# A turn in front of TensorE's first loop that jumps over the loop's code, in a chained attention and mixture-of-experts kernel

## The chip, the cores and the metric

The kernel runs on one core of a Trainium2 chip. The metric is the device time of one execution in microseconds (us). The kernel before took 394.88 us in the median of three executions (394.24 to 397.09).

## The reference

All of it is float32. Three stages stand behind one another, on 4 batches x 8 heads x 768 tokens x 48 dimensions.

```python
# 1: linear attention with decay w and bonus u, token by token
for t in range(S):
    cur = np.einsum('bhd,bhe->bhde', u[None] * kt, vt)
    y[:, :, t] = np.einsum('bhd,bhde->bhe', rt, state + cur)
    state = w[None, :, :, None] * state + np.einsum('bhd,bhe->bhde', kt, vt)
# 2: soft mixture of experts on x = y, tokens x (H*D) = 3072 x 384; 8 experts with 4 slots each
logits = x @ phi
d = softmax(logits, over tokens); slot_input = d.T @ x
slot_out[e] = relu(slot_input[e] @ w1[e]) @ w2[e]
x = softmax(logits, over slots) @ slot_out
# 3: out = relu(x @ w_in) ** 2 @ w_out, with 384 -> 2048 -> 384
```

## The kernel before, in words

The attention is cut into 24 units: 6 chunks of 128 tokens (CH = 6) by 4 pairs of heads (HP = 4), and each unit holds 4 batches. A unit is computed in matrix form: scores of keys against queries (`unit_scores`, L1005), the part of y that comes from the carried state (`unit_carried`, L1028), the part that comes from the unit's own values (`unit_own`, L1043), the step of the state (`unit_state`, L1016), the turning of the next unit's keys (`turn_keys`, L993) and of an earlier unit's x (`turn_x`, L987). The dispatch of stage 2 (`pair_logits` L973, `token_logits` L980, `turn_peaks` L1111, `spread_peaks` L1117, `gather` L1123) stands between the units' steps.

TensorE runs these units in one loop, `with pe.Fori(0, CH) as c` (L1154), whose body is written out for the 4 units of a chunk. Its order is by hand: the own part of the unit before, scores, the first half of carried, the state's step for the next unit, the second half of carried, the turning of the next keys, the turning of the x of three units ago. The other engines (VectorE is DVE, ScalarE is ACT, GpSimd is POOL, and SP issues every data transfer) have the 24 units written out without a loop. All order between engines goes by semaphores.

Ahead of the loop TensorE does this. It waits for the identity matrix and does 7 dummy products (`keep_awake`, L1130). It waits for the powers of the decay from DVE and turns them (16 small products, L1138, into `x_ps` and `kt_ps`), does 7 more dummy products, then waits for the first keys, turns them (L993) and makes the first unit's step of the state (L1016). The turned powers are needed by DVE (`kn_pow`, L729), then by POOL, which multiplies the keys with them (`keys_n`, L450), and these keys are what TensorE turns next.

Behind the loop come the experts (L1256, L1280) and then the third stage, whose products (L1320, L1340) take more than half of the time.

## Time and profile before

| | |
|---|---|
| median of three executions | 394.88 us |
| lowest, highest | 394.24, 397.09 us |
| the profiled execution | 395.28 us |
| its span, first to last instruction | 393.6 us |
| TensorE busy in the span | 382.6 us, 97% |
| VectorE, ScalarE, GpSimd busy | 250.9, 205.3, 43.9 us |
| mean granted TensorE clock | 0.991 |

The profiled execution's own time is 1.7 us longer than its span, since the span leaves out what lies ahead of the first and behind the last recorded instruction. The profile counts a busy PE by matmuls whose ends are modelled. Every float32 product that the program names once is recorded as two matmuls with two weight loads (a transpose as one of each), so a step of 16 products is a row of 32. Time in which an engine waited for nothing that the profile shows is called "issue". The queues of kind "instruction" bring the engines' own code.

### The profile page before, as it was taken

The page shows a single profiled execution, that of the slowest core. Times are in us where ns is not written, and L with a number is a line of the kernel's source. Part 1 is how long each engine was busy: PE and PEld are TensorE (multiplying, and loading weights), DVE is VectorE, ACT ScalarE, POOL GpSimd, SP SyncE. Part 2 cuts the span into 40 slices and gives each one's busy share as a digit, 9 for nine tenths or more (in the row PEclk, how much of TensorE's full clock was granted, in tenths as well). Part 3 has the DMA queues.
Part 4 walks back from the last instruction along what each step waited for, and adds up shares of the span by engine and source line. Part 5 has one row for each costly group of instructions (what it writes and reads, how often), then busy time and mean ns, then how long its engine had stood idle before and what let it go on. Part 6 is the DMA issues. An engine that isn't in the chain of part 4 may idle for free.

```text
span 393.6 us, 13159 instructions
## 1 busy us (share of the span) xinstructions
PE 382.6 (97%) x5308; PEld 337.6 (86%) x5308; DVE 250.9 (64%) x437; ACT 205.3 (52%) x378; POOL 43.9 (11%) x87
## 2 busy tenths in 40 slices
PE   7878999999999999999999999999999999999996
PEld 7667878787887533799999999999999999999996
DVE  8563887787775650498866656665666566666662
ACT  7432455655654320687665556555655565555552
POOL 7512314333310110000000000000000000000000
PEclk9996999999999999999999999999999999999999
DMA  4564799999995989800002001100200020002002
GB/s 120 179 207 159 268 300 301 295 313 299 302 358 171 378 296 408 314 0 2 0 2 80 2 0 42 38 0 0 80 0 0 0 80 0 0 0 82 0 0 82
DMA packets 29351, 50.75 MB, mean 129 GB/s; under 512 B 4112, under 2 KB 23568, under 8 KB 28944
## 3 DMA queue, kind: packets, MB, share of 16 engines
q1 hardware_dynamic: 29328, 50.44, 37.9%
q8 instruction: 14, 0.23, 0.2%
q14 instruction: 9, 0.07, 0.1%
HBM read 45.71 MB, written 4.72 MB: 128 GB/s over the span
## 4 chain that ended last, share of the span: by engine, by line
PE 96%; issue 2%; DVE 1%; DVEq 0%; ACT 0%
PE out_ps L1340 51%; PE score_ps L1005 6%; PE h_ps L1320 6%; PE y_ps L1043 4%; PE kt_ps L993 4%; PE y_ps L1028 3%; PE x_ps L987 3%; PE inc_ps L1016 3%; PE wide L1256 3%; PE wide L1280 3%; PE score_ps L973 2%; PE x_ps L980 2%; PE kt_ps L1123 1%; PE score_ps L1130 1%; PE wide L1266 1%
## 5 line engine op out<-in xcount | busy, mean ns | idle before, releaser
L1340 PE MATMUL out_ps<-w_lo,act_hi 128*128 128x384 f32 x384 | 129.1, 336 | 0.0
L1340 PE MATMUL out_ps<-w_hi,act_hi 128*128 128x384 f32 x384 | 128.7, 335 | 0.0
L1340 PE MATMUL out_ps<-w_hi,act_lo 128*128 128x384 f32 x384 | 128.3, 334 | 0.0
L945 DVE TENSOR_TENSOR act<-relu_h 128x512 f32<-128x512 f32 x96 | 66.4, 692 | 72.1 <-ACT relu_h L667 72.1
L667 ACT ACTIVATE relu_h<-h_ps 128x512 f32<-128x512 f32 x96 | 57.5, 599 | 88.8 <-PE h_ps L1320 88.8
L1340 PEld LDWEIGHTS out_ps<-w_lo,act_hi 128*128 128x128 f32 x384 | 72.0, 188 | 3.8
L1340 PEld LDWEIGHTS out_ps<-w_hi,act_hi 128*128 128x128 f32 x384 | 72.1, 188 | 0.1
L1340 PEld LDWEIGHTS out_ps<-w_hi,act_lo 128*128 128x128 f32 x384 | 72.1, 188 | 0.0
L950 DVE TENSOR_TENSOR act_lo<-act,act_hi 128x512 fp32r<-128x512 f32 x96 | 66.5, 692 | 4.6 <-ACT act_hi L670 1.0
L670 ACT ACTIVATE act_hi<-relu_h 128x512 fp32r<-128x512 f32 x96 | 60.8, 633 | 3.9
L1320 PE MATMUL h_ps<-mix_t,gin 128*128 (+1 forms) x96 | 37.5, 392 | 0.0
L520 ACT ACTIVATE keys<-kt_ps,w_inv 112x512 f32<-112x512 f32 x24 | 16.5, 687 | 28.8 <-PE kt_ps L993 27.1
L450 POOL TENSOR_TENSOR keys_n<-keys_in,kn_pow 128x384 f32<-128x384 f32 x24 | 25.3, 1053 | 54.8 <-DMA keys_in<-in_rkv_n 50.5
L1005 PE MATMUL score_ps<-queries,keys 48*64 48x128 f32 x768 | 27.8, 279 | 2.8 <-issue 2.8
L770 DVE TENSOR_TENSOR scores<-score_ps,ident_sub 128x512 f32<-128x512 f32 x24 | 16.6, 692 | 21.2 <-PE score_ps L1005 21.2
L1005 PEld LDWEIGHTS score_ps<-queries,keys 48*64 48x64 f32 x768 | 22.2, 136 | 8.0 <-issue 6.8
L1028 PE MATMUL y_ps<-queries,state_a 48*48 48x64 f32 x384 | 21.1, 223 | 0.0
L1028 PE MATMUL y_ps<-queries,state_b 48*48 48x64 f32 x384 | 20.6, 222 | 0.0
L530 ACT ACTIVATE x_t<-y_ps 112x256 f32<-112x256 f32 (+1 forms) x25 | 12.2, 486 | 14.7 <-PE y_ps L1043 14.6
L1043 PEld LDWEIGHTS y_ps<-scores,values 64*48 64x48 f32 x800 | 13.4, 122 | 6.2 <-issue 5.2
L1320 PEld LDWEIGHTS h_ps<-mix_t,gin 128*128 128x128 f32 x96 | 17.9, 188 | 0.5 <-issue 0.3
L744 DVE TENSOR_TENSOR queries<-recept,q_pow 112x512 f32<-112x512 f32 x24 | 18.3, 762 | 0.0
(173 smaller groups left out, 444.5 us busy)
## 6 DMA issues: line engine op xcount, KB each, us to landing
w_sb<-in_w SPq DMA_DIRECT2D x21, 512.0 KB, 4.9
keys_in<-in_rkv_n SPq DMA_DIRECT2D x24, 192.0 KB, 4.7
recept<-in_rk_t SPq DMA_DIRECT2D x48, 96.0 KB, 4.0
values<-in_rkv_n SPq DMA_DIRECT2D x24, 192.0 KB, 3.4
w_pre<-in_w SPq DMA_DIRECT2D x24, 192.0 KB, 5.2
w_room<-in_w SPq DMA_DIRECT2D x3, 1536.0 KB, 12.6
out_dram<-y_sb SPq DMA_DIRECT2D x5, 768.0 KB, 3.5
w_w<-in_w SPq DMA_DIRECT2D x4, 768.0 KB, 7.1
```

Source lines behind the costliest of these rows:

```text
L450: nc.gpsimd.tensor_tensor(keys_n[n % HP][:, :, :, 0:D], keys_in[n % K_BUFS][:, :, :].rearrange("p b (h d) -> p b h d", h=2), kn_pow[:, hp] ...
L667: nc.scalar.activation(relu_h[f % 2][:, :], h_ps[f % 4][:, :], ACT.Relu).then_inc(relu_done, 1)
L670: nc.scalar.activation(act_hi[f % 4][:, :], relu_h[f % 2][:, :], ACT.Square).then_inc(act_hi_done, 1)
L744: nc.vector.tensor_tensor(queries[n % Q_BUFS][0:PAIR].rearrange("p b s k t -> p (b s) k t")[:, :, 0], recept[n % R_BUFS][0:PAIR].rearrange ...
L770: nc.vector.tensor_tensor(scores[n % 2][:, :, :, :], blocks[:, :, :, 1], ident_sub[:, :].unsqueeze(1).unsqueeze(1).broadcast_to([P, 2, B, ...
L945: nc.vector.tensor_tensor(act[f % 2][:, :], relu_h[f % 2][:, :], relu_h[f % 2][:, :], ALU.mult).then_inc(act_done, 1)
L950: nc.vector.tensor_tensor(act_lo[f % 4][:, :], act[f % 2][:, :], act_hi[f % 4][:, :].bitcast(F32), ALU.subtract).then_inc(act_lo_done, 1)
L1005: last = nc.tensor.matmul(score_ps[part, at:at + P], keys[hp % 2][rows, b, part], queries[hp % Q_BUFS][rows, b, s].rearrange("p k t -> p ( ...
L1028: return nc.tensor.matmul(y_ps[head_rows(b, h), at:at + SUB], state[HEAD_ROWS[h], hp, b], queries[hp % Q_BUFS][HEAD_ROWS[h], b, s, 0], sta ...
L1043: return nc.tensor.matmul(y_ps[head_rows(b, h), at:at + SUB], values[hp][HALVES[s], b, D * h:D * (h + 1)], scores[hp % 2][HALVES[s], h, b] ...
L1320: nc.tensor.matmul(h_ps[f % 4][:, :], gin[:, P * f:P * (f + 1)], mix_t[:, bass.ds(g * B, B), :], start=True, stop=True).then_inc(h_mm, 1)
L1340: last = nc.tensor.matmul(out_ps[t][:, 0:DM], a[f % 4][:, tok], w[:, f], start=(f == 0 and i == 0), stop=(f == NF - 1 and i == 2))
```

## The change

TensorE's loop runs 7 turns, not 6. Each unit's code stands in a block that is only entered where the turn's number is over 0, so that the first turn jumps over all four. The powers' turns with the dummy products behind them are now in the loop's body, between the second and the third unit's code, in a block entered in turn 0 alone; the first unit's keys and state, and the waits that stood ahead of the loop, stand in another such block between the third and the fourth unit's code. The chunk's number, which the waits are computed from, is a register of its own that the last unit adds 1 to. What is computed is the same, and so is the order of the products within TensorE.

```diff
             pe.wait_ge(const_step, IDENT)
             keep_awake(7, score_ps)
-            pe.wait_ge(pow_t_done, 1)
...
-            last.then_inc(pow_n_done, 1)
-            keep_awake(7, score_ps)
-
-            pe.wait_ge(const_step, MASKS)
-            pe.wait_ge(kn_done, 1)
-            turn_keys(0)
...
-            with pe.Fori(0, CH) as c:
+
+            chunk = pe.alloc_register('chunk')
+            pe.reg_mov(chunk, 0)
+            with pe.Fori(0, CH + 1) as turn:
                 for hp in range(HP):
-                    n = c * HP + hp
-                    own_step(n - 1, (hp - 1) % HP)
...
+                    if hp == HP - 2:
+                        with pe.If(turn < 1):
+                            turn_powers()
                     if hp == HP - 1:
-                        pe.wait_ge(peak_read, c + 1)
...
+                        with pe.If(turn < 1):
+                            first_unit()
+                    with pe.If(turn > 0):
+                        c = pe.snap(chunk, min_val=0, max_val=CH - 1)
+                        n = c * HP + hp
+                        own_step(n - 1, (hp - 1) % HP)
...
+                        if hp == HP - 1:
+                            pe.reg_alu(chunk, chunk, 1, ALU.add)
```

`turn_powers` and `first_unit` hold, word for word, the lines that stood ahead of the loop:

```diff
+            def turn_powers():
+
+                pe.wait_ge(pow_t_done, 1)
+                for hp in range(HP):
...
+                last.then_inc(pow_n_done, 1)
+                keep_awake(7, score_ps)
+
+            def first_unit():
+
+                pe.wait_ge(const_step, MASKS)
+                pe.wait_ge(kn_done, 1)
+                turn_keys(0)
+                pe.wait_ge(ps_cleared, 1)
+                pe.wait_ge(values_in[0], 16)
+                unit_state(0)
...
```

On TensorE (PE), at the head of its program up to the loop's first products, the difference reads as follows (rows with a minus are the kernel before, with a plus the changed one).

```order
 L1130 MATMUL score_ps<-ident 128x128 x7
-L1138 MATMUL x_ps<-ident,kn_powt 64x48 x2
-L1138 MATMUL kt_ps<-ident,kn_powt 64x48 x2
...
-L1130 MATMUL score_ps<-ident 128x128 x7
-L993 MATMUL kt_ps<-ident,keys_n_70 128x128 x4
-L1016 MATMUL inc_ps<-values_81,keys_n_70 48x48 x16
-L1154 UNCONDITIONAL_BRANCH
-L1154 ISA
+L1161 UNCONDITIONAL_BRANCH
+L1169 COMPARE_AND_BRANCH
+L1170 ISA
 L1043 MATMUL y_ps<-scores_80,values_84 48x64 x16
```

The powers' turns, the dummy products behind them and the first unit are gone from here, and a compare-and-branch stands ahead of the first unit's code. The program now reaches the loop after 7 dummy products.

On PE again, at the end of the second unit's code and ahead of the third's.

```order
 L987 MATMUL x_ps<-ident,x_t 128x112 x4
+L1169 UNCONDITIONAL_BRANCH
+L1164 COMPARE_AND_BRANCH
+L1138 MATMUL x_ps<-ident,kn_powt 64x48 x2
+L1138 MATMUL kt_ps<-ident,kn_powt 64x48 x2
...
+L1130 MATMUL score_ps<-ident 128x128 x7
+L1164 UNCONDITIONAL_BRANCH
+L1169 COMPARE_AND_BRANCH
+L1170 ISA
 L1043 MATMUL y_ps<-scores_80,values_82 48x64 x16
```

Here stand the powers' turns now. In each of the 6 turns that compute, the end of the second unit meets two compare-and-branches, one of which jumps over this block.

On PE, at the end of the third unit's code and at the end of the loop's body.

```order
 L1111 MATMUL score_ps<-ident,pm 32x128 x4
+L1169 UNCONDITIONAL_BRANCH
+L1167 COMPARE_AND_BRANCH
+L993 MATMUL kt_ps<-ident,keys_n_70 128x128 x4
+L1016 MATMUL inc_ps<-values_81,keys_n_70 48x48 x16
+L1167 UNCONDITIONAL_BRANCH
+L1169 COMPARE_AND_BRANCH
+L1170 ISA
 L1043 MATMUL y_ps<-scores_79,values_83 48x64 x16
...
 L987 MATMUL x_ps<-ident,x_t 128x112 x4
-L1154 REGISTER_ALU
-L1154 COMPARE_AND_BRANCH
+L1218 REGISTER_ALU
+L1169 UNCONDITIONAL_BRANCH
+L1161 REGISTER_ALU
+L1161 COMPARE_AND_BRANCH
```

The first unit's keys and state stand ahead of the fourth unit's code, and the loop's end has one register operation and one branch more.

## Rows read from the trace of the kernel before

**Rows 1.** The page: granted clock in 40 slices, and the queue with TensorE's code.
```profile
PEclk9996999999999999999999999999999999999999
...
q8 instruction: 14, 0.23, 0.2%
```

**Rows 2.** The chain that ended last, 8 to 38 us: start us, us, what.
```profile
10.77 0.26 issue
11.03 0.67 PE y_ps L1043 x32
...
14.11 1.01 issue
15.12 0.24 PE inc_ps L1016
15.36 0.33 PE y_ps L1028 x16
15.69 0.59 PE kt_ps L993 x4
16.27 0.39 PE x_ps L987 x4
16.66 1.00 PE score_ps L973 x16
17.66 0.59 PE y_ps L1043 x32
18.26 0.96 PE score_ps L1005 x32
19.21 0.22 PE y_ps L1028 x16
19.44 0.76 issue
...
27.85 2.79 issue
...
35.93 1.04 PE y_ps L1043 x32
```

**Rows 3.** Queue q8 in 12.6:12.7, 17.7:17.8, 21.8:21.9, 28.2:28.3, 33.4:33.5 us: packets, MB, share.
```profile
q8 instruction: 1, 0.02, 60.8%
q8 instruction: 1, 0.02, 58.0%
q8 instruction: 1, 0.02, 57.9%
q8 instruction: 1, 0.02, 67.6%
q8 instruction: 1, 0.02, 62.5%
```

**Rows 4.** Windows: stretch, length, busy of PE, PEld, DVE, ACT, POOL, then PEclk, DMA share, GB/s.
```profile
30.20:37.00 6.80, 6.36 (x139) 5.79 (x143) 2.73 (x5) 0.69 (x1) 1.50 (x3) 0.50 0.50 168
```

**Rows 5.** Timeline: PE's first dummy products (of both bursts), and POOL's first keys.
```profile
1.60 3.35 PE L1130 MATMUL score_ps<-ident 128*128 128x128 f32 x14 [1.60 <-POOL ident L424]
6.46 3.35 PE L1130 MATMUL score_ps<-ident 128*128 128x128 f32 x14
7.77 2.52 POOL L450 TENSOR_TENSOR keys_n<-keys_in,kn_pow 128x384 f32<-128x384 f32 x2 [0.78 <-DVE kn_pow L729]
```

**Rows 6.** Timeline of PE around loop ends at 53.5 and 123.5 us, and at 71.4.
```profile
53.24 0.58 PE L987 MATMUL x_ps<-ident,x_t 112*128 112x112 f32 x4
53.88 0.66 PE L1043 MATMUL y_ps<-scores,values 64*48 64x64 f32 x32
...
71.43 0.67 PE L1043 MATMUL y_ps<-scores,values 64*48 64x64 f32 x32
...
123.39 0.58 PE L987 MATMUL x_ps<-ident,x_t 112*128 112x112 f32 x4
123.90 0.66 PE L1043 MATMUL y_ps<-scores,values 64*48 64x64 f32 x32
```

More of the change, by code:

```diff
@@ L1130, in keep_awake @@
                     nc.tensor.matmul(bank[:, 0:P], ident[:, :], ident[:, :], start=True, stop=True)
+            def turn_powers():
+                pe.wait_ge(pow_t_done, 1)
+                for hp in range(HP):
+                    for r, bank in enumerate((x_ps, kt_ps)):
+                        for part in HALVES:
+                            last = nc.tensor.matmul(bank[part, D * hp:D * (hp + 1)], kn_powt[HEAD_ROWS[r], hp],
+                                                    ident[HEAD_ROWS[r], HEAD_ROWS[r]], start=True, stop=True)
+                last.then_inc(pow_n_done, 1)
+                keep_awake(7, score_ps)
@@ L1135, in _ @@
-            for hp in range(HP):
-                for r, bank in enumerate((x_ps, kt_ps)):
-                    for part in HALVES:
-                        last = nc.tensor.matmul(bank[part, D * hp:D * (hp + 1)], kn_powt[HEAD_ROWS[r], hp],
-                                                ident[HEAD_ROWS[r], HEAD_ROWS[r]], start=True, stop=True)
-            last.then_inc(pow_n_done, 1)
-            keep_awake(7, score_ps)
-            pe.wait_ge(const_step, MASKS)
-            pe.wait_ge(kn_done, 1)
@@ new lines, in _ @@
+            chunk = pe.alloc_register('chunk')
+            pe.reg_mov(chunk, 0)
+            with pe.Fori(0, CH + 1) as turn:
+                for hp in range(HP):
+                    if hp == HP - 2:
+                        with pe.If(turn < 1):
+                            turn_powers()
+                    if hp == HP - 1:
+                        with pe.If(turn < 1):
[4 more added lines that the diff above has]
+                        own_step(n - 1, (hp - 1) % HP)
+                        if hp == 0:
+                            pe.wait_ge(disp_done, c + 1)
+                            pe.wait_ge(x_done, n)
+                            pe.wait_ge(k_done, n + 1)
+                            settled()
+                            gather(kt_ps)
+                        if hp == 1:
+                            pe.wait_ge(lt_done, c + 1)
+                            pe.wait_ge(lt_half, c + 1)
+                        if hp == HP - 1:
+                            pe.wait_ge(peak_read, c + 1)
+                        scores_step(n, hp)
+                        if hp in (1, 2):
+                            pe.wait_ge(y_half, c * 2 + hp)
+                        carried_step(n, hp)
+                        state_step(n + 1, (hp + 1) % HP)
+                        if hp == HP - 1:
+                            pe.wait_ge(peak_done, c + 1)
+                            pe.wait_ge(x_done, n + 1)
+                            settled()
+                            spread_peaks(x_ps)
+                        carried_rest(n, hp)
+                        if hp == 1:
+                            pe.wait_ge(x_done, n + 1)
+                            pe.wait_ge(const_step, FOLD)
+                            settled()
+                            token_logits(x_ps)
+                        if hp == 0:
+                            pe.wait_ge(slot_in_done, c + 1)
+                        keys_step(n + 1, (hp + 1) % HP)
+                        if hp == 1:
+                            pe.wait_ge(lg_free, c + 1)
+                        if hp == HP - 1:
+                            pe.wait_ge(disp_done, c + 2)
+                        turn_step(n - LAG, (hp - LAG) % HP)
+                        if hp == 0:
+                            pe.wait_ge(mask_done, n + 2)
+                            settled()
+                            pair_logits()
+                        if hp == HP - 2:
+                            pe.wait_ge(pm_done, c + 1)
+                            pe.wait_ge(mask_done, n + 2)
+                            settled()
+                            turn_peaks(score_ps[:, 0:P])
+                        if hp == HP - 1:
+                            pe.reg_alu(chunk, chunk, 1, ALU.add)
```

53 lines of the change are left out of this document (4 added, 49 removed).

## The prediction, made before the changed kernel had run

> **What bounds the kernel now.** I read the page first: TensorE is busy in all but 3% of the span, at full clock everywhere but in one slice of 40, the fourth [rows 1]. So only TensorE's time counts, and the place to look is the first 40 us. The chain of work that ended last, read in order of time there, shows what differs between the loop's first turn and the others [rows 2]. The first turn begins with the own part at 11.03 us and the second at 35.93: 24.90 us. The second turn lasts until 53.88, 17.95 us, and the third until 71.43, 17.55 us [rows 2, 6]. The first turn holds three stretches called "issue", 1.01, 0.76 and 2.79 us (4.56 us), in the middle of steps whose inputs were there; no later turn has one.
>
> What they are can be counted. From the stall at 14.11 to that at 19.44 stand 1+16+4+4+16+32+32+16 = 121 matmul records with as many weight loads, 242 instructions, and the order lists 14 waits and register operations among them: 256. From 19.44 to 27.85 the same count gives 512. TensorE's code comes in 14 packets of 0.23 MB in all, 16 KB each [rows 1], which is 256 instructions of 64 bytes. So the stalls stand at borders of code blocks, and I number the blocks so that the loop before began in block 1; the stalls are the entries to 2, 3 and 5.
>
> When is a block asked for? The packets of code start at about 12.6, 17.7, 21.8, 28.2 and 33.4 us [rows 3], and there is none before. Turns 2 to 6 fetch nothing: the program of about 3650 instructions is 15 blocks, the first two were there at the start, and 14 packets [rows 1] are the others once each with one past the end. A share of 60.8% of 16 engines in 0.1 us is a packet of 0.97 us. Each starts 1.6 to 2.8 us after the block before it was entered (15.12 to 17.7, 20.20 to 21.8, 30.64 to 33.4), and TensorE resumes 1.3 to 1.5 us after its end (13.6 to 15.12, 18.6 to 20.20). I read this as one block fetched ahead, asked for on entering the one before. From entry to the next block being there takes 4.4 us (block 1 entered at about 10.7, ahead at 15.12), 5.1 us (15.12 to 20.20), at most 4.1 for block 4 (asked for from 20.20; its border, half way to 27.85, passed without a stall), and over 6 for block 5.
>
> The longest stall has a second price: the granted clock is 0.50, the level of 1.2 GHz, from 30.2 to 37.0 us [rows 4]. The first turn is 24.90 - 17.55 = 7.35 us longer than a clean one, of which 4.56 is stall and the rest mostly this clock; the second turn has another 0.40. All that code arriving late costs before is therefore 7.75 us.
>
> **The change part by part.** *What goes.* If every block is in place when the first computing turn begins, its stalls and the clock they cost go: -7.75 us. Counting the changed order in the same way (two instructions for a matmul record with its weight load, one for each other row and wait), unit 1 to 4 begin at about 36, 376, 777 and 1161, the powers at 683, the first unit's keys at 1083, the loop's end at 1458; the borders are at 195, 451, 707, 963, 1219 and 1475. So the front turn does land in every block from 0 to 5.
>
> *What comes: the front turn's own fetches.* It needs blocks 2, 3, 4 and 5, one after the other, where nothing but the powers, dummy products and the first unit can be done meanwhile. The first dummy products start at 1.60 and take 3.35 us; the sequencer is through them at about 4.5 us [rows 5]. It jumps into block 1, which is there, and on to block 2, which is asked for only now: with the 4.1 us of the quickest fetch in the rows, block 2 is there at 8.6. The powers begin then, not at 5.4. Their last ten products stand behind the border to block 3: 12.7. POOL's first keys were ready some 2.5 us after the powers' end (the dummy products behind them start at 6.46, and half of the row at 7.77 ends at 9.03), so they are ready at 15.3, and the second 3.35 us of dummy products end at 16.1: both within the wait for block 4, which is there at 16.8. The first unit is done there; block 5 comes at 20.9, and the first computing turn begins at 21.0 instead of 11.03: +10.0 us. Bounds: a fetch that starts at once costs 1.0 for the packet and 1.3 behind it, 2.3 us, and puts the turn's start at 14.9 (+3.9); the 5.1 us of block 3 puts it at 24.9 (+13.9). I take 4.1 because it is the quickest of the fetches seen and fewer transfers are under way while the buffers are full. What is queued behind TensorE in all this: DVE's turned powers and then its scaling of queries, POOL's keys, SP's next loads of keys. All are done before 21 us, and each was ahead of TensorE before.
>
> *The clock.* TensorE idles in three stretches of up to 4 us in the front turn, more than the 2.79 us after which the clock fell before. It comes into the first turn at 1.2 GHz. How dear that is: of the 7.75 us of excess the three stalls are 4.56, so about 3.2 us were lost in the 6.8 us at half clock, 0.47 us for each. Bounds 0 (the first unit's work has warmed it) and 4.0 us (8.5 us at that rate, if the clock comes back only after more work than before). Some of the low stretch will pass while TensorE idles anyway; I take two thirds of the 3.2, 2.2.
>
> *The branches.* Each computing turn now passes nine branches instead of one. The page shows no branches, but their effect stands at the loop's ends: with the jump back taken, the own part starts 0.64 us after the x transposes (53.24 to 53.88), and without it 0.51 us (123.39 to 123.90): 0.13 us [rows 6]. The upper price is the entry to the loop, 0.26 us of issue [rows 2]. Behind the first unit 1 us of logit products covers it. Three places a turn (second unit, third, loop's end) in 6 turns: 18 x 0.13 = 2.3 us; with some register work I take 2.5, bounds 0 and 24 x 0.26 = 6.2.
>
> The Trainium skill ("Advanced Engine Details and Errata", Control Flow Timing) puts a compare-and-branch at about 108 ns; the trace's 0.13 us agrees as far as it goes. By it the 8 branches more would be 8 x 6 x 0.108 = 5.2 us if nothing covered any.
>
> *The sum*, against the profiled execution: 395.28 - 7.75 + 10.0 + 2.2 + 2.5 = 402.2 us. That execution lay 0.4 us above the median, so 401.8 us.
>
> The row shows fetches asked for one at a time [rows 3]. The Trainium skill ("Runtime: NRT & Kernel Launch", Instruction fetch mechanics) says that the sequencer fetches the next 16 KiB while it executes the present one, and that a taken branch to code that is not there stalls until it is fetched. That speaks against the change: the rule turns each of the front turn's jumps into a stall, as the sum has it. By the first half alone, with its cost "mostly hidden", the front turn would be nearly free and the sum 7.75 us less than before; the three stalls of 4.56 us in the first turn contradict it for code that runs through a block in about 4 us.
>
> **The rivals.** *Prompt fetches.* In the front turn a fetch might cost its 2.3 us alone. Block 2 at 6.8, block 3 at 9.1, then the dummy products until 12.5 cover block 4, block 5 at 14.9. For it: the packet takes only 1 us, and part of the delay ahead of it may be other transfers' load. Against: the delay is 2.6 us for the packet at 17.7 and 2.8 for that at 33.4 [rows 3], and never under 1.6. Then 395.28 + 3.9 - 7.75 + 2.5 = 393.9 with a warm clock, 393.5 against the median; if the branches hide behind products in flight too, 391.0. The first of these is no change, the second faster.
>
> *A jump that misses brings two blocks,* as two were there at the start. Then the front turn has two full waits and starts the first turn at about 17: +6.0 - 7.75 + 1.5 + 2.5, 397.1 us. For it: blocks 0 and 1 both came before the first instruction. Against: no row has a jump to code that was not there.
>
> *The code doesn't stay.* The loop now reaches from block 0 to 5 with 6 fetched behind it, seven blocks where before six stayed. If seven don't fit, each computing turn stalls at least once for 2.3 to 4.1 us: 6 x 2.3 on top of the forecast, 415 us or more. A sentence of the same section of the Trainium skill gives TensorE 2048 instructions of code memory, eight blocks, by which this does not happen; no row here shows the limit.
>
> **How the numbers follow.** The forecast, with fetches one at a time at 3.5 to 5 us, has 0.5. The two-block rival 0.15, prompt fetches with branches paid 0.15, prompt with hidden branches 0.15, code that doesn't stay 0.05. About what a measurement of this kernel can tell from no change is 1%, 3.9 us. The forecast's own range is 396 (fetches of 3.5 us, branches hidden) to 408, with a small part of it, 0.04, within 1%; together slower 0.51, within 1% 0.33, faster 0.16. The range must hold eight of ten: from 391.3, which takes in nearly all of the prompt cases, to 407.0, which leaves out the codes that don't stay and the dearest fetches with the dearest branches.
>
> **What would show it right or wrong.** In the changed trace, the queue of TensorE's code has its four packets of blocks 2 to 5 before the first own part (L1043), at about 6, 10, 14 and 18 us, and none during the first turn. The powers' products (L1138) start near 8.5 us and are split by a gap after 12 records. The first own part is at 21 us; the first turn has no issue stall and lasts 17.6 us plus the clock's part; PEclk is 0.50 at its start. The later turns are 17.55 + 0.4 us. The prediction is wrong if the packets follow each other in 2.5 us (own part near 15), if two packets come in a pair, or if the turns stay at 17.55 us, and badly so if packets come in later turns.

## The result, and the profile of the changed kernel

The changed kernel takes 400.99 us, the median of 4 runs (400.71 to 401.74), beside 395.25 us (394.24 to 397.09, 4 runs) for the kernel before on the same chip: a ratio of 1.0143, 95% interval 1.0102 to 1.0184. It is slower by 5.7 us. The profiled executions are 400.90 and 395.28 us, their spans 399.1 and 393.6, and all of the 5.5 us between the spans is there when the loop ends: the last own part begins at 129.41 us, before at 123.90 [rows 6].

The page of the changed kernel answers to [rows 1]:

```profile
PEclk9889999999999999999999999999999999999999
...
q8 instruction: 14, 0.23, 0.2%
```

There are as many packets of code as before. The stretch at a lower clock has moved from the fourth slice of 40 to the second and third. What each packet of code answers is seen in PE's timeline of the front turn (start us, length us, engine, line, operation; in brackets the idle time ahead and what ended it):

```profile
5.86 0.34 PE L1138 MATMUL x_ps<-ident,kn_powt 48*64 48x48 f32 x2 [0.91 <-DVE kn_powt L717]
...
9.61 0.34 PE L1138 MATMUL kt_ps<-ident,kn_powt 48*64 48x48 f32 x2 [3.08 <-issue]
...
10.41 3.26 PE L1130 MATMUL score_ps<-ident 128*128 128x128 f32 x14
13.87 0.63 PE L993 MATMUL kt_ps<-ident,keys_n 128*128 128x128 f32 x4 [0.19 <-POOL keys_n L450]
14.42 0.57 PE L1016 MATMUL inc_ps<-values,keys_n 64*48 64x48 f32 x32
18.88 0.42 PE L1043 MATMUL y_ps<-scores,values 64*48 64x64 f32 x5 [3.89 <-issue]
```

and in the queue of code in 3.0:3.1, 7.3:7.4, 10.9:11, 15.6:15.7 and 18.7:18.8 us, which answers to [rows 3]:

```profile
q8 instruction: 1, 0.02, 80.0%
...
q8 instruction: 1, 0.02, 63.2%
...
q8 instruction: 1, 0.02, 77.4%
...
q8 instruction: 1, 0.02, 60.2%
...
q8 instruction: 1, 0.02, 68.2%
```

Blocks 2, 3, 4 and 5 come one at a time, 3.6 to 4.7 us apart, and the packet at 18.7 is block 6, asked for as block 5 was entered; from 18.9 to 130 us the queue has no packet. The powers stop at the border to block 3 and wait 3.08 us. Block 4 (packet at 10.9) is nearly hidden behind the dummy products: only 0.19 us of idle time is left. Block 5 (packet at 15.6) has nothing in front of it, 3.89 us of idle time.

The two brackets that name another engine mislead. The trace also holds records of TensorE's branches, with start and length, which the views above leave out. The jump to block 2 stands at 2.36 us and takes 3.31, to 5.67 us, 0.3 us after DVE is through with the powers' input (5.37). The jump to block 4 stands at 9.88 and takes 3.69, to 13.57 us, and the keys are turned 0.30 us later. In the kernel with three wide dummy products below that jump ends at 13.84, and the keys are turned 0.30 us later again. So all four fetches are waited for, one after the other, until the jump to block 5 (at 15.03, 2.90 us) ends at 17.93. The loop's end and the first unit's header then take 0.9 us more, and the first own part starts at 18.88, where before it stood at 11.03 [rows 2].

The chain of waits shows the same end of the front turn (start us, us, what):

```profile
14.49 0.51 PE inc_ps L1016 x32
15.00 3.89 issue
18.88 1.10 PE y_ps L1043 x32
```

The own part takes 1.10 us here and 0.67 at full clock [rows 2]. The windows say why (columns as in rows 4):

```profile
16.86:23.69 6.83, 4.81 (x96) 3.45 (x100) 0.28 (x1) 1.21 (x2) 1.05 (x2) 0.50 0.31 92
23.70:38.40 14.70, 14.67 (x508) 12.69 (x500) 10.95 (x21) 5.57 (x10) 4.84 (x7) 1.00 0.53 165
```

From 16.86 to 23.69 us the granted clock is 0.50, 1.2 GHz. It comes after 1.9 us of the last wait and lasts 4.8 us into the first turn; the rest of that turn has TensorE busy in 14.67 of 14.70 us. So the three stalls of the first turn are gone, as the change's shape promised.

The turns' lengths, from own part to own part, tell the rest:

| Turn | 1 | 2 | 3 | 4 | 5 | 6 |
|---|---|---|---|---|---|---|
| before, us | 24.86 | 17.99 | 17.55 | 17.53 | 17.53 | 17.44 |
| changed, us | 19.51 | 18.53 | 18.20 | 18.27 | 18.22 | 17.83 |
| difference | -5.35 | +0.54 | +0.65 | +0.74 | +0.69 | +0.39 |

These sum to -2.34, and with the front turn's 18.85 - 11.00 = +7.85 us they make the 5.5. (The starts here are those of the own part's first weight load, up to 0.04 us ahead of its first product.) The 0.54 is counted against a second turn that still had 0.44 us of late code and low clock in it; 0.3 us of the changed kernel's second turn is a wait for DVE (`logits_t`, L762), which the kernel before does not have. At the end of a turn, around 56 us, PE's timeline answers to [rows 6]:

```profile
55.99 0.57 PE L987 MATMUL x_ps<-ident,x_t 112*128 112x112 f32 x4
56.92 0.66 PE L1043 MATMUL y_ps<-scores,values 64*48 64x64 f32 x32 [0.35 <-issue]
```

0.93 us from transposes to own part, before 0.64 us from 53.24 to 53.88: the group of transposes ends, and TensorE has nothing to issue for 0.35 us.

### The profile page after: what moved, and what is told of

It is laid out like the page before. It is cut to its first block, busy times and chain, and to the rows that moved or that the text cites. A ratio compares the mean times of both kernels' runs of the same rounds, so it can differ in the third digit from the quotient of the medians.

```text
span 399.1 us, 13266 instructions
## 1 busy us (share of the span) xinstructions
PE 383.2 (96%) x5308; PEld 336.7 (84%) x5308; DVE 250.3 (63%) x437; ACT 205.3 (51%) x378; POOL 42.8 (11%) x87
## 4 chain that ended last, share of the span: by engine, by line
PE 92%; issue 4%; POOL 2%; DVE 1%; DVEq 0%; ACT 0%; POOLq 0%
PE out_ps L1357 50%; PE score_ps L1005 6%; PE h_ps L1337 6%; PE y_ps L1043 4%; PE kt_ps L993 3%; PE inc_ps L1016 3%; PE y_ps L1028 3%; PE x_ps L987 3%; PE wide L1273 3%; PE wide L1297 3%; PE kt_ps L1123 2%; PE score_ps L973 2%; PE x_ps L980 2%; PE wide L1283 1%; PE wide L1317 1%
## 5 line engine op out<-in xcount | busy, mean ns | idle before, releaser
L1005 PEld LDWEIGHTS score_ps<-queries,keys 48*64 48x64 f32 x768 | 21.9, 136 | 5.8 <-issue 4.8
L1043 PE MATMUL y_ps<-scores,values 64*48 64x64 f32 x800 | 17.0, 224 | 5.7 <-issue 5.3
```

The source lines that it names most:

```text
L1005: last = nc.tensor.matmul(score_ps[part, at:at + P], keys[hp % 2][rows, b, part], queries[hp % Q_BUFS][rows, b, s].rearrange("p k t -> p ( ...
L1043: return nc.tensor.matmul(y_ps[head_rows(b, h), at:at + SUB], values[hp][HALVES[s], b, D * h:D * (h + 1)], scores[hp % 2][HALVES[s], h, b] ...
```

## Experiments

All kernels are compared with the kernel before, run beside them on the same chip. The theory: the front turn costs one fetch a block, one after the other, less what work covers; a low clock follows it; and the branches cost in every turn. The rivals: a jump brings two blocks; the branches are free and the later turns are longer for another reason; the first turn is long for the front turn's order, not the clock.

**The branches alone.** All conditional blocks stay, but the powers and the first unit stand ahead of the loop again, which begins at turn 1.

```diff
+            turn_powers()
+            first_unit()
             chunk = pe.alloc_register('chunk')
             pe.reg_mov(chunk, 0)
-            with pe.Fori(0, CH + 1) as turn:
+            begin = pe.alloc_register('begin')
+            pe.reg_mov(begin, 1)
+            with pe.Fori(pe.snap(begin, min_val=0, max_val=1), CH + 1) as turn:
```

> The changed loop with its conditional blocks, but entered at turn 1: the powers' turns and the first unit stand ahead of it again, so there is no front turn (dead copies of the two blocks stay in the loop). Theory (the three accounts: code waits moved to the front about even, clock 1.3 us, branches about 4 us): turns 3 to 5 take 18.2 us as in the changed kernel, the first turn keeps its stalls at the borders of code blocks, and the time is before + 4, about 399 us. Rival (the longer turns come from the front turn or from where the code lies, not from the branches): turns of 17.55 us and about 395 us.

Measured: 400.25 us (400.08 to 401.25), ratio 1.0150 (1.0079 to 1.0221). The waits of PE in the first 56 us (us in total, times, longest) show that the stalls are back:

```profile
PE y_ps L1028 <- issue: 2.4, 2, 1.6
...
PE y_ps L1043 <- issue: 1.5, 2, 1.1
PE inc_ps L1016 <- issue: 1.1, 1, 1.1
PE x_ps L987 <- issue: 1.0, 1, 1.0
```

and the third and fourth turns last 18.31 and 18.32 us, 0.77 more than 17.55 and 17.53. The branches cost what they cost without any front turn. With them alone the kernel is as slow, to 0.7 us, as with the front turn too, so by the medians the front turn takes about as much as it gives. (By the terms added up below it takes 1.9 us more. Two things hide that here: the first turn is 1.0 us longer than before's, and the first own part stands 0.7 us later, most of it because the keys and the state ahead of it ran slowly, 1.06 and 0.79 us for 0.66 and 0.57.)

**The front turn without conditional branches.** The path is the changed kernel's (into the loop's code, over the units, to the powers, the first unit, the loop's end), made of unconditional jumps around three pads. (A pad is a piece of code that stands inside the loop's body and is reached by a jump from in front of the loop; each turn jumps over it.)

```diff
+            ahead = nc.cur_bb
+            pe.br('pad_powers')
+            nc.switch_bb('to_loop', parent=ahead)
...
+                    if hp == 2:
+                        here = nc.cur_bb
+                        pe.br('unit_2')
+                        nc.switch_bb('pad_powers', parent=ahead)
+                        turn_powers()
+                        pe.br('pad_first')
+                        nc.switch_bb('unit_2', parent=here)
```

The pads of the first unit (ahead of the fourth unit) and of the loop's end are written likewise.

> The same front path (first dummies, a landing in block 2 with the powers, block 4 with the first unit, block 5, back to the loop's head), but by unconditional jumps; the loop has its 6 turns and no conditional blocks, only one jump over each of three pads. Theory: the first own part near 18.9 us as in the changed kernel, turns of 17.6 to 17.8 us, the time 3 to 3.5 us under the changed kernel's, about 397.5 us: still not faster than before, since what the front turn waits for (7.8 us) is what the first turn's stalls cost. Rival (the branches are not it): turns of 18.2 us and 401 us. If a jump past a block brings two blocks in a pair, the own part is nearer 15 us and the time under 394 us.

Measured: 397.81 us (396.78 to 398.1), ratio 1.0072 (1.0038 to 1.0106); one of ten executions took 622.0 us with a mean granted clock of 0.556, where the others have 0.987 to 0.996; what lowered it I don't know. The packets of code start at 2.59, 6.70, 10.01, 14.32 and 18.52 us: still one at a time, though the jumps here go straight to code that is not there. No pair comes, so "a jump that misses brings two blocks" falls. The first own part is at 18.39 us, as late as in the changed kernel:

```profile
7.29 0.26 PE L1138 MATMUL x_ps<-ident,kn_powt 48*64 48x48 f32 x2 [2.42 <-DVE kn_powt L717]
8.91 0.34 PE L1138 MATMUL x_ps<-ident,kn_powt 48*64 48x48 f32 x2 [1.17 <-issue]
...
18.39 0.47 PE L1043 MATMUL y_ps<-scores,values 64*48 64x64 f32 x8 [3.65 <-issue]
```

The third and fourth turns last 17.79 and 17.80 us, 0.25 over before's, with three jumps a turn: unconditional jumps cost a third of what the branches do. The powers' input from DVE is 1.9 us late here; more on this below.

**Work in front of the last wait, many products.** To tell the clock's part from the rest, dummy products fill the wait for block 5: 14 small ones behind the first unit.

```diff
                 unit_state(0)
+                keep_awake(14, score_ps)
                 pe.wait_ge(ps_cleared, 3)
```

> The changed kernel with 14 more dummy products behind the first unit's state, into the scores' bank, which fill TensorE's idle time while block 5 is fetched. Theory: the sequencer waits for block 5 either way, so the first own part stays at 18.9 us or moves by under 0.5 us, the clock is full in the first turn, that turn takes 18.2 instead of 19.5 us, and the time falls by 1.3 us to 399.7 us. Rival (the first turn's 1.3 us are not the clock): 401 us or more, as the dummy products only add work.

Measured: 403.38 us (401.93 to 404.6), ratio 1.0224 (1.0146 to 1.0302). The expectation was missed, and for a reason of this kernel's own: the 56 instructions pushed the loop's end over the border at 1475 into block 6. Up to the first own part there are now six packets, at 3.0, 6.9, 10.8, 15.5, 18.6 and 21.7 us. The fifth is block 6, and the wait for it stands in PE's timeline (the sixth is the block behind it):

```profile
17.30 1.39 PE L1130 MATMUL score_ps<-ident 128*128 128x128 f32 x11
21.84 0.41 PE L1043 MATMUL y_ps<-scores,values 64*48 64x64 f32 x10 [3.15 <-issue]
```

As a test of the clock it says nothing, since the clock is 0.50 again from 22.05 to 25.46 us. But it prices a block by itself: one more on the front turn's way puts the first own part 3.0 us later (21.84 for 18.88), although dummy products had been added for cover.

**The same with few instructions.** Three products of 512 columns in about that place: twelve instructions, by the count of two for a record with its weight load, where the 14 small ones were 56.

```diff
                 pe.wait_ge(lt_done, 1)
+                for i in range(3):
+                    nc.tensor.matmul(score_ps[:, 0:BANK], ident[:, :], logits_t[:, :, :], start=True, stop=True)
                 pe.wait_ge(params_in, 4 * 16)
```

> The changed kernel with 3 dummy products of 512 columns behind the first unit's state (12 instructions instead of the 56 of the run before, which moved the loop's end over the border into block 6, so that the front turn had one fetch more). They keep TensorE busy for about 2.6 us of its idle time before block 5 is there. Theory: the first own part stays at 18.9 us, since five packets are fetched as before; the clock stays full or falls for less, the first turn takes 18.2 to 19 us and the time is 399.7 to 400.5 us. Rival (the first turn's 1.3 us are not the clock): 401 us, the first turn 19.5 us.

Measured: 398.73 us (398.63 to 399.76), ratio 1.0084 (1.0060 to 1.0107). PE's timeline and a window of the first turn:

```profile
17.03 1.02 PE L1154 MATMUL score_ps<-logits_t,ident 128*128 128x512 f32 x2
19.79 0.67 PE L1043 MATMUL y_ps<-scores,values 64*48 64x64 f32 x32 [1.74 <-issue]
```

```profile
13.90:36.00 22.10, 20.06 (x616) 15.53 (x620) 12.12 (x23) 7.76 (x13) 6.40 (x13) 1.00 0.55 170
```

The clock stays at 1.00, the own part takes 0.67 us, and the first turn lasts 17.46 us, not 19.51, in the same code. The low clock therefore costs 2.05 us, more than the 1.3 expected, and all of it is in the first unit (5.36 us for 7.44; the other three agree within 0.06 us). It is no accident of one execution: the mean granted clock is 0.999 to 1.000 in all four of this kernel and 0.983 to 0.991 in all four of the changed one. The own part comes 0.9 us later than expected, at 19.79: the packet of block 5 is longer here, 1.85 us for 0.96. The time is 1 us under the expected 399.7 to 400.5. The branches still cost (turns 3 and 4: 18.19 and 18.39 us).

**What the front turn is good for, without its price.** If the fetch needs only a visit, a visit can be short. Here the order ahead of the loop is before's, and the sequencer is sent to pads of one wait (already fulfilled) and a jump back: to block 2 behind the first dummy products, to block 3 behind the powers and the second ones, and to block 4 from the end of the first unit in every turn, each time with products still queued.

```diff
             keep_awake(7, score_ps)
-            pe.wait_ge(pow_t_done, 1)
...
+            ahead = nc.cur_bb
+            pe.br('pad_2')
+            nc.switch_bb('front_1', parent=ahead)
+            turn_powers()
+            pe.br('pad_3')
+            nc.switch_bb('front_2', parent=ahead)
+            first_unit()
...
+                    if hp == 2:
+                        here = nc.cur_bb
+                        pe.br('unit_2')
+                        nc.switch_bb('pad_3', parent=ahead)
+                        pe.wait_ge(const_step, IDENT)
+                        pe.br('front_2')
+                        nc.switch_bb('unit_2', parent=here)
```

> The powers' turns and the first unit stand ahead of the loop as before; the sequencer makes short detours to one-instruction pads in the loop's code while dummy products are queued: to block 2 during the first seven, to block 3 during the second seven, and from the end of each turn's first unit, under the logit products, to block 4, so that block 5 is asked for early. Theory (a fetch costs nothing where the engine has queued work): blocks 2 and 3 arrive at about 5.7 and 9.4 us, powers 0.4 us later than before, first own part near 11.4 us, no stall in the first turn, full clock, turns at most 0.2 us longer: 395.3 + 0.4 - 7.75 + 1 = about 389 us. Rival (a detour drops what was fetched or the fetches serialise with the start): the stalls of the first turn stay or the own part starts at 14 us or later, 395 us or more.

Measured: 390.35 us (389.44 to 391.47, 10 runs), ratio 0.9888 (0.9856 to 0.9921). In the profiled execution the clock is full in every turn; the mean granted clock of the ten is 0.994 to 1.000. The turns last 17.31, 17.82, 17.55, 17.54, 17.69 and 17.45 us: no stall, and no price for four jumps a turn (0.16 to 0.17 us each by their records from the second turn on). The start was expected at 11.4 us and is at 13.53:

```profile
7.55 0.35 PE L1138 MATMUL x_ps<-ident,kn_powt 48*64 48x48 f32 x2 [2.60 <-DVE kn_powt L717]
...
13.53 0.67 PE L1043 MATMUL y_ps<-scores,values 64*48 64x64 f32 x32 [0.16 <-issue]
```

The powers begin at 7.55 us, 5.42 before, because DVE had its weights late. In DVE's timeline of this kernel the copy of the weights stands at

```profile
5.31 0.29 DVE L711 COPY w_pow<-w_sb 112x4 f32<-112x4 f32 x1 [2.05 <-DMA w_sb<-in_w_t]
```

Before, this copy is at 3.31 us. The transfer that it waits for is one of the first that SP issues, and the first packet of code, at 3.18 us, falls among them. The packet's time alone doesn't decide it: in the changed kernel it is at 3.0 us, and the copy stands at 3.31.

**Two variants of it.** With the pads of blocks 2 and 3 alone, the first detour held back until POOL's fourth step (`pe.wait_ge(const_step, 4)` ahead of it):

```diff
+            pe.wait_ge(const_step, 4)
             ahead = nc.cur_bb
             pe.br('pad_2')
...
                     if hp == 1:
                         here = nc.cur_bb
-                        loop_bb = here
-                        pe.br('pad_4')
+                        pe.br('unit_1')
...
-                    if hp == 3:
-                        here = nc.cur_bb
-                        pe.br('unit_3')
...
```

> Detours to block 2 and block 3 in front of the loop only, none to block 4 from the first unit's end; the first detour waits for the fourth constant, some 0.6 us later than in the run with all pads. Theory: blocks 2, 3 and 4 are there in time, block 5 is asked for only when block 4 is entered near 22 us and takes 3.1 to 6 us: a stall of 0 to 2 us in the fourth unit, 389 to 391 us. Rival (block 4 must be visited to be there): stalls in the third unit too, 393 us or more.

Measured: 392.75 us (390.28 to 394.58, 9 runs), ratio 0.9953 (0.9914 to 0.9992). The expected 389 to 391 us was missed by the median. The profiled execution is the quickest, 390.28 us, and its chain of waits has no idle time in the first turn. The median is 2.05 us above that of the next kernel, which has all pads and ran beside it on the same chip. The three executions with a mean granted clock of 0.999 or more take 390.28 to 391.38 us, the other six (0.995 or 0.996) 391.07 to 394.58. So something lets the clock fall in most of them; whether block 4 or 5 comes late there, without a pad of its own, one profile can't say. With all pads and the first detour held back, the edit to the first kernel with pads is one line:

```diff
+            pe.wait_ge(const_step, 4)
             ahead = nc.cur_bb
             pe.br('pad_2')
```

> All three pads, with the first detour held back until POOL's fourth constant is there (about 2.2 us). Theory: in the run with all pads the code fetch asked for at 1.7 us stood among SP's first transfers and let the decays land at 5.3 instead of 3.3 us, so that the powers came 2.1 us late; asked for at 2.3 us as in the changed kernel, the decays land at 3.3, the powers start near 5.9, the first own part near 11.5 and the time is 388.3 us. Rival (the decays' lateness is chance or comes from any early fetch): the powers again at 7.5 us, 390.3 us.

Measured: 390.70 us (389.93 to 390.93), ratio 0.9876 (0.9851 to 0.9902); expected were some 2 us less. DVE's copy is at 3.30 us again, but the powers are no earlier for it:

```profile
7.04 0.34 PE L1138 MATMUL x_ps<-ident,kn_powt 48*64 48x48 f32 x2 [2.09 <-issue]
```

The detour is asked for later and comes back later, and TensorE waits for it by itself: the jump stands at 2.21 us and takes 4.52, with its packet at 4.39, where in the first kernel with pads it stood at 1.66 and took 3.88. Holding it back moved the wait from DVE to the sequencer. In these two placements the fetch ahead of the powers costs 2.1 and 1.6 us; in the changed kernel, with the jump at 2.36, it cost 0.44. Why a packet is there at 3.0 us in one case and at 4.39 in the other is left open.

**No fetch ahead of the powers.** The first pad (block 2) is visited behind the powers and the second dummy products; the pads of block 3 and 4 are visited in every turn from the end of the first and of the second unit.

```diff
+            turn_powers()
+            ahead = nc.cur_bb
+            pe.br('pad_2')
+            nc.switch_bb('front_2', parent=ahead)
+            first_unit()
...
+                    if hp == 1:
+                        here = nc.cur_bb
+                        loop_bb = here
+                        pe.br('pad_3')
+                        nc.switch_bb('pad_2', parent=ahead)
+                        pe.wait_ge(const_step, IDENT)
+                        pe.br('front_2')
+                        nc.switch_bb('unit_1', parent=here)
+                    if hp == 2:
+                        here = nc.cur_bb
+                        mid_bb = here
+                        pe.br('pad_4')
+                        nc.switch_bb('pad_3', parent=loop_bb)
+                        pe.wait_ge(const_step, IDENT)
+                        pe.br('unit_1')
+                        nc.switch_bb('unit_2', parent=here)
...
+                        nc.switch_bb('pad_4', parent=mid_bb)
+                        pe.wait_ge(const_step, IDENT)
+                        pe.br('unit_2')
```

> No fetch before the powers: one detour in front of the loop, to block 2 during the second seven dummy products, and in every turn a detour to block 3 from the end of the first unit and to block 4 from the end of the second. Theory: powers at 5.4 us and the first own part at 11.1 us as before; block 2 is asked for near 6 and there near 10, block 3 follows at 14, block 4 by the first detour near 20, block 5 by the second near 25; no stall, but the uncovered detour costs 0.1 to 0.2 us in each turn: 388 to 389.5 us. Rival: the later chain misses block 4 or 5 by a microsecond or two, 390 to 392 us.

Measured: 390.03 us (389.52 to 391.71), ratio 0.9877 (0.9843 to 0.9911). The expected 388 to 389.5 us was missed by half a microsecond. The powers are at 5.41 us, the first own part at 11.27, and the first turn lasts 17.68 us at full clock. The jump to block 2 ends at 9.62 us and is waited for:

```profile
10.03 0.63 PE L993 MATMUL kt_ps<-ident,keys_n 128*128 128x128 f32 x4 [2.18 <-issue]
```

In later turns the second unit takes 4.66 us for 4.59 and the third 3.82 for 3.75. With the pad of block 4 left out:

```diff
                     if hp == 2:
                         here = nc.cur_bb
-                        mid_bb = here
-                        pe.br('pad_4')
+                        pe.br('unit_2')
                         nc.switch_bb('pad_3', parent=loop_bb)
...
-                    if hp == 3:
-                        here = nc.cur_bb
-                        pe.br('unit_3')
...
```

> As the run with one detour in front, but without the detour to block 4 from the second unit's end: block 2 in front, block 3 from the first unit's end, block 5 asked for when block 4 is entered. Theory: the first own part at 11.2 us, no stall of a microsecond or more, since in the run with two pads block 5 was asked for just as late and no stall showed; the turns lose the 0.05 to 0.1 us at the second and third unit's ends: 389.5 to 390 us. Rival (block 5 is late as in the kernel before): a stall of 1 to 3 us in the fourth unit, 391 to 393 us.

Measured: 389.87 us (387.96 to 392.22), ratio 0.9860 (0.9787 to 0.9933), the lowest median of the study, though not one that can be told from the 390.03. In PE's timeline the wait for block 2 stands ahead of the first unit, as in the kernel just before it:

```profile
10.00 0.63 PE L993 MATMUL kt_ps<-ident,keys_n 128*128 128x128 f32 x4 [2.14 <-issue]
10.56 0.58 PE L1016 MATMUL inc_ps<-values,keys_n 64*48 64x48 f32 x32
11.24 0.67 PE L1043 MATMUL y_ps<-scores,values 64*48 64x64 f32 x32
```

The start is before's, 11.24 for 11.03 us, and five of the six turns last 17.45 to 17.99. The first lasts 18.74 us, and the low clock is in its first unit (6.85 us for 5.46 in the kernel just before):

```profile
11.80:15.21 3.41, 3.41 (x55) 2.14 (x52) 0.33 (x1) 1.39 (x3) 0.80 (x2) 0.50 0.60 173
```

The wait isn't enough to explain that: the kernel just before idles 2.18 us in the same place, and its profile has no low clock. Of the four executions of each, two have a mean granted clock of 0.999 or more and two of 0.994 to 0.996. So the low clock comes in some executions of either kernel.

The first kernel with pads, the one held back and these two start at 13.5, 13.0, 11.3 and 11.2 us, and their medians lie within 0.9 us of each other. Waits for DVE are a part of why: the waits of PE from 28 to 124 us, of the variant with the detour held back,

```profile
PE score_ps L1005 <- DVE logits_t L762: 1.6, 3, 0.7
```

where the kernel before has no wait on `logits_t`; the other three have 0.4 to 0.9 us of them. Part of what an earlier start gives is lost to inputs that come later than TensorE wants them.

**The unit's header alone.** What in the conditional blocks costs: the kernel before, with each unit in a block whose condition always holds, no blocks of turn 0 and no second counter.

```diff
+            bound = pe.alloc_register('bound')
+            pe.reg_mov(bound, CH)
+            limit = pe.snap(bound, min_val=1, max_val=CH)
             with pe.Fori(0, CH) as c:
                 for hp in range(HP):
-                    n = c * HP + hp
...
+                    with pe.If(c < limit):
+                        n = c * HP + hp
```

> The kernel before with each unit's code in a conditional block that is always entered: four untaken branches and four recomputed chunk numbers a turn, no front turn, no blocks jumped over, no register for the chunk. Against the run with all the branches (turns of 18.31 us against 17.54) it tells the headers from the two skipped blocks and the second counter. Theory (a branch that isn't taken is 0.07 us, a taken one 0.21, by their records): the headers give 0.2 to 0.35 us a turn, the time 1.5 to 2 us over before, 396.5 us. Rival (the headers are all of it): turns of 18.3 us, 399.5 us.

Measured: 396.50 us (393.21 to 398.66, 10 runs), ratio 1.0032 (0.9993 to 1.0071). The median can't be told from no change, but it is the expected one, and the trace resolves it: at a turn's end 0.26 us of idle time,

```profile
71.03 0.67 PE L1043 MATMUL y_ps<-scores,values 64*48 64x64 f32 x32 [0.26 <-issue]
```

where the changed kernel has 0.34 and 0.35; turns 3 to 5 last 17.94 us, 0.40 more than before, a little over the 0.2 to 0.35 expected. So about half of the 0.77 us a turn is the units' headers, the other half the two skipped blocks and the second counter. TensorE's records of branches give the sizes: a compare-and-branch that is not taken (a unit's header) 0.07 us, one that is taken (over a skipped block, or back to the loop's start) 0.21, each plus the register operations beside it.

## Why the prediction came out right, step by step

The forecast was 401.8 us: 395.28 - 7.75 + 10.0 + 2.2 + 2.5, less the 0.4 us by which the profiled execution lay above the median. The changed kernel took 400.99. The four terms, measured in the spans:

| Term | predicted | measured | from |
|---|---|---|---|
| front turn | +10.0 | +7.85 | first own parts 11.00 and 18.85 |
| late code gone | -7.75 | -7.99 | 24.86 - 17.31 in turn 1, 17.99 - 17.55 in turn 2 |
| clock | +2.2 | +2.05 | turn 1: 19.51, with the clock full 17.46 |
| branches | +2.5 | +3.60 | the rest: 17.46 - 17.31 in turn 1, then 0.98, 0.65, 0.74, 0.69, 0.39 |
| sum | +6.95 | +5.51 | |

The 17.31 us of a clean first turn is that of the first kernel with short pads. The branches' term is what is left over; 0.3 us of it is the wait for DVE in turn 2. Two terms were mis-sized, by -2.15 and +1.10 us, in opposite directions, so the sum, 1.4 us off, came nearer than the larger of them: that much of the hit is luck.

*One block at a time, asked for on entering the one before.* Right: five packets, none in a pair, none up to the loop's end, in this kernel and in the one with jumps. It was the step on which the sign hung. "Prompt fetches" (own part near 15 us) fell with it: the packets are 3.6 to 4.7 us apart, not 2.5. The trace of before had the delay ahead of a packet in it [rows 3], while a packet's 1 us alone would have promised a gain.

*The front turn, +10.0: 2.15 us too much.* The step that failed is "the sequencer is through them at about 4.5 us". It had been read from the end of the dummy products [rows 5], but the first packet of code is at 3.0 us: the jump to block 2 is recorded at 2.36 us. The sequencer had run ahead of the products it had queued, and asked for block 2 while they ran. The Trainium skill ("TensorE: Matmul & The Clock Gate", Architectural detail) gives TensorE a queue of 64 instructions, and the 28 of the first dummy products fit in it; no run here shows the depth. So block 2 was there at 5.67 us, not at 8.6, and held the powers up by only 0.44 us (5.86 for 5.42). That this wait was the fetch's, and not DVE's as the view has it, shows in three kernels with the same code up to there: with DVE through at 5.36 or 5.37 us in each, and the packet of block 2 lasting 1.28, 1.40 and 1.64 us from 3.0 us on, the powers start at 5.86, 5.97 and 6.21. The later fetches, taken at 4.1 us each, were right: the jumps show blocks 2 and 5 there at 5.67 and 17.93 us, 12.26 us apart for three fetches, 12.3 forecast. That keys and dummy products would end within block 4's wait was right too. The way from block 5's arrival to the first own part had been taken at 0.1 us and is 0.9: the loop's end, its branch back and the first unit's header. So the term is -2.9 us at its head and +0.8 at its tail.

*Late code gone.* Right to 0.3 us, and so was the place of the borders: the powers split behind their thirteenth record (predicted: twelfth), the first unit is in block 4, the loop's end in block 5. The kernel with 14 more dummy products showed the border at 1475 by crossing it.

*The clock.* Right in size: 2.05 us for 2.2, by the one kernel in which the loop is the same and the clock stays full. The rate came from [rows 4]; the two thirds of it were a guess, which the trace bears out (TensorE busy in 4.81 of the 6.83 us at 0.50). The prediction's "full clock everywhere but in one slice" was read off the page and is wrong for the first microseconds, as the last section shows; no term hung on it.

*The branches, +2.5: 1.1 us too little.* The step that failed is "0.13 us a place". It was read from one compare-and-branch that is taken, at the loop's end [rows 6]. By their records taken ones last 0.21 to 0.22 us, in the kernel before too, so the 0.13 was at best the part of one that showed. The end of a turn now has the end of the fourth unit's block, the second counter's addition, the loop's own branch and the first unit's header in a row, and they add up: +0.39 to 0.48 us there, against 0.11 to 0.16 at the ends of the second and third units. Behind the first unit the cost is 0 (5.26 us before and after), as forecast, since logit products are in flight. Nor are there nine branches a turn: the trace has seven records, three taken of 0.21 us and four not taken of 0.07, together 0.68 us more than before's single one, beside the 0.65 to 0.74 us by which turns 3 to 5 are longer. The Trainium skill's 108 ns for a compare-and-branch ("Advanced Engine Details and Errata", Control Flow Timing) fits neither: TensorE's records have 0.07 us not taken and 0.21 taken, and the measurement decides. The headers alone cost 0.30 us at the loop's end (4.24 us for 3.94) and 0.10 behind the third unit (3.85 for 3.75). How much of a branch the products in flight cover at each place was not measured by itself.

*The code stays.* Right: from 18.9 us to the loop's end not one packet of code, with seven blocks in place by then. In the kernel with 14 more dummy products there are eight (the last packet at 21.7 us, the next only behind the loop), and they stay too. What would happen with nine, no run shows.

## What to carry to other kernels

A stall called "issue" in a stretch whose inputs were ready, at equal counts of instructions in the first pass of a loop and never again, was code that arrives late here; count 256 instructions from one to the next and look at the queue of code before believing it. The name beside an idle time can be wrong for the same reason: two waits for code stood under DVE's and POOL's name, since the view knows of no event that ends a fetch. A visit does fetch code ahead, but only one block a visit and some 4 us each, so the visits belong where products or waits for data are under way: a jump to a pad of one fulfilled wait and a jump back does this for 0 to 0.07 us in a later turn and took 1.1 to 1.4% off this kernel (0.5% with the two visits ahead of the loop alone), while a whole empty turn, with conditions around every unit, pays for its fetches in a row and for the conditions in every turn. Count where such a detour puts the loop's end too: 56 instructions over a border cost 3 us.

## What the runs showed of the hardware that was not expected

- A fetch of code early in the program disturbs other transfers, or they it. In the changed kernel two loads of `recept` take SP 2.25 us to issue, from 2.38 us on, while the first packet of code is at 3.0. In SP's timeline:

```profile
2.38 2.25 SPq L340 DMA_DIRECT2D recept<-in_rk_t  x2
```

  Before, the same row has 0.90 us. It has 2.38 and 2.62 us in the two kernels with more dummy products (packets at 3.0) and 1.87 in the one with jumps (2.59). With the first detour held back (packets at 4.24 and 4.39 us) the long issue is a later one, the two loads of `recept` at 4.27 us: 1.82 and 1.88 us for 0.89. So in six kernels the long issue moves with the first packet. In the kernel with jumps and the first with pads (packets at 2.59 and 3.18 us) DVE's copy L711 comes about 2 us late, for want of its weights. That the late weights have the same cause is argued from the times and was not tried by itself.
- TensorE's sequencer runs well ahead of the products: it jumps at 2.36 us in the changed kernel and at 1.66 in the one with jumps, and the packets are there at 3.0 and 2.59, while the first dummy products run until 4.95.
- Unconditional jumps, 0.16 us each by their records, cost nothing at the ends of the second and third units: these take 4.59 and 3.75 us in the kernel with jumps, as before, and only at the loop's end, where it holds one too, a unit takes 4.16 to 4.22 us for 3.94. The kernel with pads has none there and turns of 17.55 and 17.54 us.
- TensorE starts at its lower level, 1.2 GHz, whatever the granted clock of a view says. The views read 1.00 for the first microseconds of every run, but the seven first dummy products take 3.27 to 3.36 us in all of them. The seven second ones, the same products, take 3.35 us before, in the first kernel with pads, and in the kernel with jumps, where the granted clock is given as 0.50; in the two kernels without a fetch ahead of the powers they take

```profile
6.03 1.83 PE L1130 MATMUL score_ps<-ident 128*128 128x128 f32 x14
```

  So the clock comes up near 5 us in some executions and only after the second dummy products in others, even with the same code up to there (the powers' first products take 0.34 us in the changed kernel and 0.26 in the one with 14 more dummy products).
- Where it had come up early it could fall again: in the kernel with jumps it is 0.50 from 8.05 to 14.88 us, after 2.42 and 1.17 us of idle time. In the first kernel with pads the 2.60 us of idle time ahead of the powers stand before the clock had come up at all. Of two profiles that idle 2.14 and 2.18 us in the same place, the clock falls in one. What decides is left open.
